# Four-corner products for queries and state sums, and values scaled on GpSimd, in a delta-rule attention kernel with two feed-forward layers

## The reference

```python
# attention with the delta rule, state is 48x48 for each of 32 heads
k_n = k / (norm(k) + 1e-6)
for t in range(768):
    y[t] = q[t] @ state
    v_old = state.T @ k_n[t]
    state = state + beta[t] * outer(k_n[t], v[t] - v_old)
# first feed-forward layer, 3072 tokens x 384, inner width 2048
h = x @ w_in;  x2 = maximum(0.01 * h, h) @ w_out
# 8 experts, inner width 1024, one expert per token
e = argmax(x2 @ w_gate + modality_bias[modality_id]);  gate = softmax(...)[e]
out = gate * (maximum(x2 @ w1[e], 0) @ w2[e])
```

## Time and profile before

| | us |
|---|---|
| median of 3 runs (977.09 to 982.07) | 978.0 |
| the profiled execution | 978.93 |
| its span, first to last instruction | 977.2 |
| PE busy | 870.9 |
| DVE busy | 553.5 |
| ACT busy | 350.6 |
| POOL busy | 87.6 |

### The profile page before, as it was taken

One profiled execution on the slowest core, in us unless ns is written; L12 is line 12 of the kernel. 1 busy time (PEld: TensorE's weight loads), 2 busy tenths in 40 slices (PEclk: granted clock), 3 DMA queues, 4 the chain that ended last, 5 costly groups with the idle time before them and its releaser, 6 DMA issues.

```text
span 977.2 us, 26906 instructions
## 1 busy us (share of the span) xinstructions
PE 870.9 (89%) x10528; PEld 766.0 (78%) x10529; DVE 553.5 (57%) x1578; ACT 350.6 (36%) x609; POOL 87.6 (9%) x100
## 2 busy tenths in 40 slices
PE   3775889989999998999989999999969999999962
PEld 3664678878888887888878888888759898889862
DVE  4974994588638862798359842344642333333350
ACT  3364335542545253444444342323411212121230
POOL 1000000000020002000100001010121212121210
PEclk9965899999999999999999999999999999999996
DMA  9904272345143533344153313255051111111122
GB/s 127 337 4 75 62 150 68 68 107 101 34 92 74 104 62 52 99 86 81 41 102 84 74 28 84 58 94 175 32 171 33 48 32 48 32 48 32 40 74 73
DMA packets 148308, 77.92 MB, mean 80 GB/s; under 512 B 112496, under 2 KB 144240, under 8 KB 147824
## 3 DMA queue, kind: packets, MB, share of 16 engines
q1 hardware_dynamic: 143264, 66.59, 30.4%
q0 software_dynamic: 4096, 9.48, 3.2%
q10 hardware_dynamic: 848, 0.39, 0.2%
HBM read 59.30 MB, written 13.21 MB: 74 GB/s over the span
## 4 chain that ended last, share of the span: by engine, by line
PE 67%; DVE 15%; ACT 7%; DMA 4%; issue 3%; SPq 1%; ACTq 1%; DVEq 0%; POOL 0%; POOLq 0%
PE bank L518 17%; PE bank L503 14%; PE bank L605 11%; PE bank L580 10%; DVE inv_t L1299 2%; DVE inv_tmp L1293 2%; PE bank L590 2%; PE bank L381 2%; PE bank L410 2%; ACT diag L987 2%; DVE g_raw L1368 1%; PE bank L484 1%; DVE tr L1305 1%; PE bank L471 1%; DVE inv_a L1255 1%
## 5 line engine op out<-in xcount | busy, mean ns | idle before, releaser
L518 PE MATMUL bank<-wo_hi,g_hi 128*128 128x392 f32 x384 | 139.1, 362 | 7.3 <-DVE g_lo L1373 4.0
L518 PE MATMUL bank<-wo_hi,g_lo 128*128 128x392 f32 x384 | 132.2, 344 | 0.0
L518 PE MATMUL bank<-wo_lo,g_hi 128*128 128x392 f32 x384 | 132.1, 344 | 0.0
L1368 DVE SCALAR_TENSOR_TENSOR g_raw<-g_raw 128x512 f32<-128x512 f32 x96 | 66.3, 691 | 105.0 <-ACT g_raw L1043 105.0
L503 PE MATMUL bank<-x_hi,wi_hi 128*128 128x512 f32 x288 | 118.3, 411 | 6.2 <-ACT g_raw L1043 3.4
L1043 ACT ACTIVATE g_raw<-bank 128x512 f32<-128x512 f32 x96 | 57.3, 597 | 170.5 <-PE bank L503 170.1
L503 PE MATMUL bank<-x_hi,wi_lo 128*128 128x512 f32 x288 | 114.0, 396 | 0.0
L503 PE MATMUL bank<-x_lo,wi_hi 128*128 128x512 f32 x288 | 113.9, 395 | 0.0
L1050 ACT ACTIVATE g_hi<-g_raw 128x512 fp32r<-128x512 f32 x96 | 60.7, 632 | 116.9 <-DVE g_raw L1368 116.9
L1373 DVE TENSOR_TENSOR g_lo<-g_raw,g_hi 128x512 fp32r<-128x512 f32 x96 | 66.3, 691 | 41.9 <-ACT g_hi L1050 41.7
L518 PEld LDWEIGHTS bank<-wo_hi,g_hi 128*128 128x128 f32 x384 | 72.7, 189 | 13.8 <-issue 6.0
(11 more groups left out here) (215 smaller groups left out, 1493.3 us busy)
## 6 DMA issues: line engine op xcount, KB each, us to landing
wo_lo<-wo_lo_d SPq DMA_DIRECT2D x80, 196.0 KB, 2.4
w_raw<-in_moe_w SPq DMA_DIRECT2D x6, 1536.0 KB, 8.4
x_rows<-stage SPq DMA_DIRECT2D x6, 770.0 KB, 6.2
kq_in_rows<-in_k SPq DMA_DIRECT2D x6, 768.0 KB, 7.0
k_raw<-in_k SPq DMA_DIRECT2D x24, 192.0 KB, 4.0
vals<-in_v SPq DMA_DIRECT2D x48, 96.0 KB, 2.9
kq_in_rows<-in_q SPq DMA_DIRECT2D x6, 768.0 KB, 8.8
x_raw<-y_t SPq DMA_DIRECT2D x33, 96.0 KB, 2.4
```

What stands on the lines that cost most here:

```text
L518: mm = pe.matmul(acc[i][:, 0:DX], g[f % 2][:, P * i:P * i + P], w, start=(f == 0 and k == 0), stop=(f == FT - 1 and k == 2))
L1368: dve.scalar_tensor_tensor(out=g_raw[f % 2][:], in0=g_raw[f % 2][:], scalar=0.01, in1=g_raw[f % 2][:], op0=ALU.mult, op1=ALU.max).then_inc ...
```

## The change

- `gram_q` and `state_sum` fill two banks in a call, for even and odd pairs, with all four corners in use. `gram_q(t, c)` is called twice a set, in slot 15 (chunk 0, of the next set) and slot 0 (chunk 1), and waits until all four banks of queries are drained. `state_sum(t, c)` is called twice, in slot 7 behind `down` and in slot 12 ahead of it.
- On DVE `mask_q` and `add_s` take an odd bank in two instructions of 64 partitions each, since its halves are swapped. `add_s` of chunk 1 stands ahead of `norm` (and, in the first round, of `split_x(0)`).
- `scale_v` moves from DVE's slot 5 to POOL, where it stands ahead of clearing `inv_t` and runs when the values and the norms are there.
- `merge_x` and `merge_p` of chunk 1 move behind `down` of their slots. `copy_p` stays.
- `old_values` of chunk 0 moves from slot 5 to slot 4, behind `down`; its `sub_w` moves in slot 5 ahead of `copy_x` and `rest_g`.

```diff
-            def gram_q(t, m):
-                for i in range(2):
-                    pe.wait_ge(*is_drained(("QT", t, m % 2 * 2 + i)))
-                b, done = fill(("QK", t, m))
+            def gram_q(t, c):
+                for m in range(4):
+                    pe.wait_ge(*is_drained(("QT", t, m)))
+                to = [fill(("QK", t, c, odd)) for odd in range(2)]
                 for j in range(8):
-                    pair = m % 2 * 8 + j
-                    for hh in range(2):
-                        mm = pe.matmul(b[half_p(hh), CH * j:CH * j + CH], k_t[head_p(hh), pair, chunk(m // 2)],
-                                       q_t[head_p(hh), pair, chunk(m // 2)], start=True, stop=True)
-                mm.then_inc(done, 1)
+                    for odd in range(2):
+                        for hh in range(2):
+                            mm = pe.matmul(to[odd][0][half_p(hh ^ odd), CH * j:CH * j + CH], k_t[head_p(hh), 2 * j + odd, chunk(c)],
+                                           q_t[head_p(hh), 2 * j + odd, chunk(c)], start=True, stop=True)
+                        if j == 7:
+                            mm.then_inc(to[odd][1], 1)
...
-            def state_sum(t, c, m):
-                if c == 0 and m == 0:
+            def state_sum(t, c):
+                if c == 0:
                     pe.wait_ge(s.k_in, 64 * t + 64)
...
+                to = [fill(("S", t, c, odd)) for odd in range(2)]
...
                 if cur:
-                    if f < 3:
-                        gram_q(n + 1, f + 1)
+                    if f == 0:
+                        gram_q(n + 1, 1)
                     if f == 5:
                         merge_x(n + 1, 0)
-                        merge_x(n + 1, 1)
                     if f == 6:
                         merge_p(n + 1, 0)
-                        merge_p(n + 1, 1)
...
                     if f == 12:
-                        state_sum(n + 1, 1, 0)
+                        state_sum(n + 1, 1)
...
                 if cur:
-                    if f == 5 and n >= 0:
+                    if f == 4 and n >= 0:
                         old_values(n + 1, 0)
+                    if f == 5:
+                        merge_x(n + 1, 1)
+                    if f == 6:
+                        merge_p(n + 1, 1)
                     if f == 7:
-                        state_sum(n + 1, 0, 0)
-                        state_sum(n + 1, 0, 1)
-                    if f == 12:
-                        state_sum(n + 1, 1, 1)
+                        state_sum(n + 1, 0)
...
-            for t in range(1, SETS):
-                pool.wait_ge(s.tt_ready, t)
-                pool.memset(inv_t[:], 0.0).then_inc(s.tm_zero, 1)
-                if t == 2:
+            def scale_v(t):
+                pool.wait_ge(s.v_in, 128 * t + 128)
+                pool.wait_ge(s.den_rdy, t + 1)
+                pool.tensor_tensor(vals[:], vals[:], den_s[:].unsqueeze(2).broadcast_to([P, GROUPS, HD]), ALU.mult
+                                   ).then_inc(s.vals_rdy, 1)
+
+
+            for n in range(-1, TT - 1):
+                scale_v(n + 1)
+                if is_set(n + 2):
+                    pool.wait_ge(s.tt_ready, n + 2)
+                    pool.memset(inv_t[:], 0.0).then_inc(s.tm_zero, 1)
+                if n == 1:
                     pool.wait_ge(s.list_out, 16)
-                if t >= 2:
-                    scatter_ids(t - 2)
+                if n >= 1:
+                    scatter_ids(n - 1)
...
+            def halves(odd):
+                return [(half_p(hh), half_p(1 - hh)) for hh in range(2)] if odd else [(slice(0, P), slice(0, P))]
+
+            def mask_q(t, c, odd):
+                dve.wait_ge(*is_filled(("QK", t, c, odd)))
+                for to, at in halves(odd):
+                    mm = dve.tensor_tensor(qk_t[to, every_other(c, odd), :], by_8(att_bank(("QK", t, c, odd))[at, :]),
+                                           mask[at, :].unsqueeze(1).broadcast_to([to.stop - to.start, 8, CH]), ALU.mult)
+                mm.then_inc(drain(("QK", t, c, odd)), 1)
...
+            def add_s(t, c, odd):
+                dve.wait_ge(*is_filled(("S", t, c, odd)))
+                old, new = state[c], state[1 - c]
+                for to, at in halves(odd):
+                    mm = dve.tensor_tensor(new[to, odd::2, :], old[to, odd::2, :], by_48(att_bank(("S", t, c, odd))[at, :]), ALU.add)
+                mm.then_inc(drain(("S", t, c, odd)), 1)
...
                 if cur:
-                    if f < 3:
-                        mask_q(n + 1, f + 1)
+                    if f == 0:
+                        mask_q(n + 1, 1, 0)
+                        mask_q(n + 1, 1, 1)
                     if f == 5:
+                        if n >= 0:
+                            sub_w(n + 1, 0, 0)
+                            sub_w(n + 1, 0, 1)
                         copy_x(n + 1, 0)
...
                 if nxt and f == 15:
-                    mask_q(n + 2, 0)
+                    mask_q(n + 2, 0, 0)
+                    mask_q(n + 2, 0, 1)
...
                     if f == 5:
                         copy_x(n + 1, 1)
-                        scale_v(n + 1)
-                        if n >= 0:
-                            sub_w(n + 1, 0, 0)
-                            sub_w(n + 1, 0, 1)
...
+                if cur and f == 12:
+                    add_s(n + 1, 1, 0)
+                    add_s(n + 1, 1, 1)
                 if nxt:
...
                         norm(n + 2)
-                if cur and f == 12:
-                    add_s(n + 1, 1, 0)
-                    add_s(n + 1, 1, 1)
```

More of the change, by code:

```diff
@@ L466, in state_sum @@
                     pe.wait_ge(*is_drained(("U", t, c, odd)))
-                b, done = fill(("S", t, c, m))
+                to = [fill(("S", t, c, odd)) for odd in range(2)]
                 for j in range(8):
[L469 to L473, removed]
+                    for odd in range(2):
+                        g = PAIRS * c + 2 * j + odd
+                        for hh in range(2):
+                            mm = pe.matmul(to[odd][0][head_p(hh ^ odd), HD * j:HD * j + HD], k_raw[half_p(hh), g, :], u_sb[half_p(hh), g, :],
+                                           start=True, stop=True)
+                        if j == 7:
+                            mm.then_inc(to[odd][1], 1)
             def outputs(t, c):
                 for m in range(2):
-                    pe.wait_ge(*is_drained(("QK", t, 2 * c + m)))
+                    pe.wait_ge(*is_drained(("QK", t, c, m)))
                     pe.wait_ge(*is_drained(("U", t, c, m)))
@@ L1334, in sub_w @@
                 dve.tensor_tensor(x, x, by_48(att_bank(("W", t, c, odd))), ALU.subtract).then_inc(drain(("W", t, c, odd)), 1)
-            def add_s(t, c, m):
-                dve.wait_ge(*is_filled(("S", t, c, m)))
-                old, new = (state[i][:, eight(m), :].rearrange("p a b -> p (a b)") for i in (c, 1 - c))
-                dve.tensor_tensor(new, old, att_bank(("S", t, c, m))[:, 0:8 * HD], ALU.add).then_inc(drain(("S", t, c, m)), 1)
+            def add_s(t, c, odd):
[4 more added lines that the diff above has]
+                mm.then_inc(drain(("S", t, c, odd)), 1)
             def split_wi(p):
```

## The result

| | before | after |
|---|---|---|
| median, us | 977.55 (4 runs, 977.07 to 982.07) | 991.75 (4 runs, 989.55 to 995.45) |
| ratio after / before | | 1.0146, 95% interval 1.0110 to 1.0182 |
| again, beside experiments 5 to 8 | 991.15 (13 runs) | 1002.68 (4 runs), ratio 1.0128 (1.0087 to 1.0170) |
| span of the profiled execution | 977.2 | 987.8 |

Slower by 1.3 to 1.5%. "The first group" is that of the first row. One run of the kernel before beside experiments 5 to 8, of 1023.35 us at a lower clock, is left out of the ratios.

A forecast was written before the change was run, and what follows sets the result against it. DVE was taken as nearly as much the bound as PE in slots 13 to 4, PE alone in 6 to 12; 978.9 - 1.3 (without Pool) + 17.4 (Pool's hold) - 3.5 (absorbed) - 0.9 (to median) = 990.6, stated 990; own range 984 to 998.

The forecast's parts named there:

- The query wait: Slot 15: gram_q of chunk 0 waits 3 us for ACT's copies of query banks 2 and 3, down(15) queued behind.
- Round 0 is full on DVE throughout: ... 0: Round 0: +1.2 us before `tr` and -1.2 behind it, so no net change apart from Pool and clock.
- Values scaled by Pool: Pool's 2.9 us scaling amid the inverse holds DVE its whole length in six sets: +17.4, less 3.5 absorbed.
- x_lo's shape ... inside the -0.7, not beside it: Slot 5: scale_v leaving DVE, 1.76 us by x_lo's shape, counts inside the -0.7 behind `tr`, not as extra saving.
- DVE as the bound from norm to `tr`: From norm to the end of `tr`, DVE works 43.16 of 47.65 us, nearly as much the bound as PE.
- -1.7 each: Rounds 2, 3 and 4 each 1.7 us shorter, from -0.5 at `tr`, -0.7 behind it and -0.5 in slot 7.
- Start: Before the first tile: masks +1.2 us and add_s ahead of split_x(0) some 1.5 late, +2.7 (0 to +5).
- PE's clock: Behind the 3 us wait in slot 15 PE's clock drops: +0.5 us in each of four rounds (0 to 1.5).
- no hindrance: Rival: Pool and DVE don't hinder each other while Pool scales; about 977 us, chance 0.32.
- sharing: Rival: DVE runs at half rate for 2.9 us beside Pool, +6.5, about 983 us; chance 0.17.
- PE's gain in full: Rival: DVE follows and all that PE is spared counts; about 950 us, chance 0.05 for it in large part.
- 6.3 a round: PE's saving in each round from gram_q, state sums and two removed waits, if PE were the only bound.

The follow-up runs named there:

- experiment 5: The kernel before, unchanged, profiled on the second chip: 993.32 us (one run).
- experiment 6: The kernel after, unchanged, on the second chip: 1002.68 us, ratio 1.0128 to before.
- experiment 7: The kernel after, but Pool's scaling starts when DVE has done the inverse's last two-input step: 993.21 us, ratio 1.0036 to before.
- experiment 8: First run of the combined kernel, on the second chip: 979.49 us, ratio 0.9897 to before.
- experiment 9: The kernel before with only gram_q and mask_q in four corners: 996.54 us, ratio 1.0061 to before.
- experiment 1: The kernel after with scale_v back on DVE, in slot 5 ahead of sub_w: 999.45 us, ratio 1.0135 to before.
- experiment 11: The combined kernel with the scaling on DVE in slot 5, ahead of sub_w: 991.18 us, ratio 1.0016 to before.
- experiment 12: The combined kernel again, unchanged, on the third chip: 981.53 us, ratio 0.9917 to before.
- combined kernel: The kernel after with queries as before, Pool's scaling behind the inverse, first-round add_s behind norm: 979.49 and 981.53 us, ratios 0.9897 and 0.9917.
- experiment 4: The kernel before with only scale_v moved to Pool, run once values and norms are there: 1001.02 us, ratio 1.0162 to before.
- experiment 10: The combined kernel with Pool scaling the values as soon as they are there: 989.41 us, ratio 0.9996 to before.
- experiment 2: The kernel after with chunk 0's gram_q behind down(15) and the next tile's up: 1001.3 us, ratio 1.0144 to before.
- experiment 3: The kernel after with gram_q and mask_q as before, in slots 15, 0, 1, 2: 989.47 us, ratio 1.0063 to before.

## Why the prediction was right, and where only its sum was

Forecast 990, ratio 1.012 to 1.013; measured 991.75, 1.0146, and 1.0128 in experiment 6. Direction and both mechanisms stood; the sizes of several terms did not, and that the total came out so close is in part luck, since their errors cancel. By the start of the first `up` of each tile, in the two profiled executions of the first group, and in those of experiments 6 and 5, which share a chip:

| stretch | on record, Pool's hold in it | measured, first group | experiment 6 less 5 |
|---|---|---|---|
| start, to tile 0 | 2.7 + 2.9 = 5.6 | 4.1 | 5.4 |
| round 0 | 0 + 0.5 + 2.9 - 0.7 = 2.7 | 7.7 | 6.1 |
| round 1 | -0.9 + 0.5 + 2.2 = 1.8 | 0.6 | -0.9 |
| rounds 2, 3, 4 | 1.0, 1.0, 0.5 | -1.3, 1.0, -0.2 | -0.3, 2.4, -0.1 |
| sum | 12.6 | 12.0 | 12.7 |

(The clock's 0.5 stands in rounds 0 to 3, which have a `gram_q` in slot 15. The experts give 1.4 back: the spans of the first group differ by 10.6. Its medians differ by 14.2; 3.6 of that is not in the two executions profiled, of which that of before is above its median and that of after the fastest of four.)

- **The query wait** was forecast as 3 us in slot 15 from ACT's order. In rounds 1 to 3 it is 3.03, 2.99 and 2.98. By the walk, from the norm to the start of `down(15)` is 14.6; from 414.25 to 428.88 it is 14.6. This step held to the tenth of a us, in those rounds.
- **The step that failed is "Round 0 is full on DVE throughout: ... 0".** I knew that x comes late over SP at its end and used that only to halve round 1. But the new wait stands behind `split_x`, which waits for that x; 4.32 in this profile, 5.89 in experiment 6, 5.76 in experiment 9, with the lower level of the clock behind it (0.52 and 0.50 over 6 us in the first and the last). The walk had been made for one round with an early x and was taken for the round with the late one. Round 0 against before (experiment 5), all on one chip, takes the 0 apart: 3.5 shorter with neither the queries nor Pool's early start (experiment 8), 1.4 longer with the queries (experiment 7), 6.1 longer with Pool at once too (experiment 6). So the queries cost 4.9 there, and 7.2 when they are the only edit (experiment 9), Pool's place 4.7 where the record has 2.2, and the rest gives 3.5 back where the record has nothing.
- **Values scaled by Pool**: +17.4 less 3.5 on record. The duration was 2.77 where I took 2.9 (bounds 1.76 and 4.4). Held by whole instructions: shown. Mis-sized is what the hold costs: the whole length was taken in every set, but in sets 2, 3 and 4 of the kernel after Pool fell beside three masks, which it doesn't hold, and 8.6 us were held in all. Experiment 7 gets back 9.5, so 13.9 was too much by some 4. That it is more than what was held (8.7 in experiment 6) is not explained by a row; the clock may have a part in it. Between 100 and 660 the granted clocks of 5 us windows put some 60 us at the lower level in experiment 6 and 44 in experiment 7; 16 us at half speed are worth at most 8, an estimate. The estimate in the prediction from the Trainium skill (GPSIMD Engine Reference, section 3), 3.4 for the operation, was too long against 2.77.
- **"x_lo's shape ... inside the -0.7, not beside it"**: in the kernel after nothing shows this wrong, but experiments 1 and 11 do: with old values in slot 4 and `sub_w` ahead of `copy_x`, 1.74 us more in slot 5 cost 9.7 in all (experiment 11 against 12), 6.6 of it seen as that wait. What Pool's scaling was for was not PE time or DVE time, but the bank that `merge_x` waits for.
- **DVE as the bound from norm to `tr`.** On record 45.7 (47.65 before). For sets 3, 4 and 5 it is 48.4, 48.4 and 51.1 in the kernel after, with Pool out of the way (experiment 7) still 49.4, 49.0 and 48.0, and in the combined kernel 46.2 each (47.6 before). So `add_s` ahead of the norm seems to shorten it, by 1.4; in experiment 7, which differs from the combined kernel of the same chip by the queries and the first `add_s`, that and more is given back. The six masks and PE's slow start behind the wait are the likely reason, not separately shown. I had the stretch shrinking by 2 despite them; "-1.7 each" for rounds 2 to 4 was too good. Experiment 7 against 5 has -0.1, 0.0 and -3.1 for them.
- **Start**: +2.7 (0 to +5), by `add_s` ahead of `split_x`. The first `up` of tile 0 is 4.1 late in the kernel after, 3.6 in experiment 7 and 0.4 in the combined kernel, where `add_s` stands behind again (experiments against 5): the right cause, about 1 too cheap. For Pool's hold in set 0 the record has 2.9 more. It costs 0.0 in experiment 4 and 0.3 in experiment 10 against 12, though 1.9 lie between experiments 6 and 7.
- **PE's clock**: +0.5 in a round. The first `down` behind the wait has 3.71 instead of 2.13: 1.6; what the end of the round keeps of it was not measured by itself.
- The rivals: no hindrance (977) is refuted by held operations, sharing (983) by their form, and PE's gain in full (950) by slot 15. Part of that gain exists nonetheless: in rounds 0 to 4 the combined kernel is 3.5, 1.6, 3.3, 2.5 and 1.8 shorter than before on its chip. Two slips of the record's sums decide nothing: the terms of its 6.3 a round add up to 6.2, and its sign "102.8 + 0.5" leaves out the clock's 0.5 of the sum. From first `up` to first `up`, round 3 takes 103.8 after and 102.7 before.

The change is thus a group of parts that gains as a whole (the four-corner state sums, `add_s` ahead of the norm from round 0 on, the split merges and the early old values) and two parts that were put in the wrong place: the four-corner queries tie the first product to the last copy, and Pool's scaling was right but a stage too early. Left open is what makes up the 1.62% of experiment 4, some 16 us: operations are held by 14.3 in all, of which the 2.6 of set 0 don't show in the start, while experiment 10 loses only 7.9 for 14.0 held. The clock drop of the next section may be the rest: in experiment 4's profile it adds 7.0 in the five rounds against that of before in the first group, but the before of its own chip was not profiled.

## What to carry to other kernels

A product that fills more banks in one call can wait for more inputs, as `gram_q` does here: walk its last input back to the DMA in every round, the first above all, since the round with the late transfer pays for it, and again in the clock behind it. GpSimd's multiply was free here only beside DVE's transposes and its products of PSUM with one tile: choose its start by what DVE does then, not by when its data is there. And when a part looks free to undo, ask which bank or buffer another part of the same change now hangs on it.

## What the runs showed of the hardware

- Pool's two-input multiply of 128x1536 fp32 takes 2.77 us. A DVE cast of 8 columns from SBUF to SBUF is held like a two-input operation (2.77 instead of 0.17).
- The kernel before takes 977.6, 984.6, 991.2 and 990.2 in the medians of four groups of runs, the last three on three chips; within one group its runs still spread by 5 to 12 us. Two of its profiles differ by 14.4 us in the span, and 9.1 of it lie where the clock differs. Behind `merge_x` of round 2 PE works without a break in both, with the same instructions in the same order. First the one of experiment 5 (`merge_x`, then two stretches), then the one of the first group, in the same order:

```profile
352.49 2.21 PE L419 MATMUL bank<-tr,inv_s 32*32 32x32 f32 x128 [1.10 <-DVE tr L1305]
```

```profile
354.00:356.00 2.00, 2.00 (x51) 1.96 (x44) 1.96 (x4) 1.17 (x2) 0.00 (x0) 0.73 0.03 8
356.00:358.00 2.00, 2.00 (x8) 2.00 (x7) 1.92 (x4) 1.95 (x3) 0.00 (x0) 0.50 0.00 0
```

```profile
346.91 2.21 PE L419 MATMUL bank<-tr,inv_s 32*32 32x32 f32 x128 [1.11 <-DVE tr L1305]
```

```profile
348.00:350.00 2.00, 2.00 (x77) 1.96 (x70) 1.95 (x4) 0.75 (x2) 0.00 (x0) 1.00 0.04 8
350.00:352.00 2.00, 2.00 (x53) 1.75 (x53) 1.94 (x3) 1.98 (x2) 0.00 (x0) 1.00 0.00 0
```

The clock falls to 0.50 in one and stays at 1.00 in the other, behind 128 records of 32x32 and a wait of 1.1. In the first it falls so in every round, and from the `up` of slot 5 to that of slot 6 each takes 1.5 us more (3.0 in round 0). In experiment 9, which leaves the merges as they were, three of the five rounds have the drop and two have not. In none of the kernels with the merges on both sides of `down` and the scaling on Pool (after, experiments 2, 3, 6, 7, 8, 10 and 12) do rounds 1 to 4 lengthen there: 6.9 in each profile. Whether splitting the merges keeps the clock was not tested by itself.
